# One routing step per slot in the last two heads, its list ahead of the drain's logits, and three output tiles behind the first expert pass

## What is computed

```
attn = softmax(scale * q @ k.T + bias);  x = attn @ v            # (2304, 512)
noisy = x @ w_gate + log1p(exp(x @ w_noise)) * noise             # (2304, 8)
top2, top2_w = best two experts of a token, softmax of their two logits
out[token] = sum over its 2 experts e of  w * (relu(x @ w1[e]) @ w2[e])
```

## Time and profile before

| what | value |
|---|---|
| median of 3 runs | 810.96 us (809.89 to 811.56) |
| the profiled execution | 811.59 us |
| its span, first to last instruction | 809.7 us |
| PE busy | 765.8 us (95%) |
| DVE busy | 495.8 us (61%) |
| ACT busy | 391.5 us (48%) |
| POOL busy | 383.4 us (47%) |
| granted TensorE clock, mean | 0.983 |

### The profile page before, as it was taken

The page is one execution under the profiler, slowest core; times in us unless marked ns, Lnnn a source line. Parts: engine busy times, 40 slices in busy tenths (PEclk is TensorE's granted clock), DMA queues, the critical chain, the costliest instruction groups (busy, mean ns, idle before and its releaser), DMA issues.

```text
span 809.7 us, 18522 instructions
## 1 busy us (share of the span) xinstructions
PE 765.8 (95%) x6658; PEld 623.7 (77%) x6658; DVE 495.8 (61%) x1233; ACT 391.5 (48%) x835; POOL 383.4 (47%) x440
## 2 busy tenths in 40 slices
PE   4886999999999998998999999999999999999994
PEld 2335676776776665978898998998998988988983
DVE  5997898998998897865536335235344344353310
ACT  5996787887887776414324133233232232242200
POOL 0007899899899783063333324314413413423312
PEclk9996999999999999998999999999999999999998
DMA  7785343353353273227633714804804705613112
GB/s 169 214 229 134 107 132 102 104 163 106 107 158 103 87 235 123 63 70 270 189 113 64 204 73 75 253 11 78 260 13 76 249 15 102 221 38 54 39 27 39
DMA packets 51575, 98.49 MB, mean 122 GB/s; under 512 B 12720, under 2 KB 21552, under 8 KB 51504
## 3 DMA queue, kind: packets, MB, share of 16 engines
q1 hardware_dynamic: 39920, 74.55, 29.6%
q0 software_dynamic: 10720, 22.72, 14.0%
q10 hardware_dynamic: 864, 0.29, 0.2%
HBM read 66.38 MB, written 20.53 MB: 107 GB/s over the span
## 4 chain that ended last, share of the span: by engine, by line
PE 80%; DMA 6%; DVE 5%; ACT 3%; issue 3%; POOL 1%; another core or an unknown queue 1%; ACTq 0%; SPq 0%; POOLq 0%; DVEq 0%
PE ps L765 27%; PE po L779 22%; PE po L677 11%; PE ps L595 8%; PE pt L622 6%; DMA out_rows<-ys,iscat 2%; PE pt L601 2%; ACT work L1308 2%; DMA slab<-work 2%; PE pt L636 1%; ACT work L1289 1%; DVE ohlo L1054 1%; PE pt L609 1%; DMA qraw<-in_qT 1%
## 5 line engine op out<-in xcount | busy, mean ns | idle before, releaser
L765 PE MATMUL ps<-xT,whi 128*128 128x320 f32 (+1 forms) x960 | 164.4, 310 | 1.6 <-ACT xT L1458 0.9
L779 PE MATMUL po<-whi,hT 128*128 128x512 f32 x640 | 159.9, 395 | 0.0
L765 PEld LDWEIGHTS ps<-xT,whi 128*128 128x128 f32 x960 | 145.8, 189 | 2.7 <-issue 2.2
L1469 ACT ACTIVATE hT<-ps 128x320 fp32r<-128x320 f32 x112 | 48.8, 437 | 200.8 <-PE ps L765 181.3
L1232 DVE SCALAR_TENSOR_TENSOR hT<-ps,hT 128x320 fp32r<-128x320 f32 x112 | 54.9, 492 | 137.8 <-ACT hT L1469 119.0
L779 PEld LDWEIGHTS po<-whi,hT 128*128 128x128 f32 x640 | 118.2, 188 | 24.6 <-DVE hT L1077 0.5
L1532 POOL TENSOR_SCALAR work<-work,rcp 128x576 f32<-128x576 f32 (+1 forms) x160 | 117.7, 745 | 26.1 <-DVE rcp L947 25.7
L1572 POOL DMA_INDIRECT xg<-x_rows,igath x38 | 42.3, 1112 | 178.5 <-DVE ys L1247 78.8
L934 DVE CUSTOM_DVE_ANT_0 ns<-ps,slab 128x576 f32<-128x576 f32 (+1 forms) x160 | 119.8, 750 | 10.1 <-PE ps L595 6.4
L1324 ACT ACTIVATE work<-ns,nmax 128x576 f32<-128x576 f32 (+1 forms) x160 | 123.1, 769 | 3.9 <-DVE nmax L934 3.8
L1585 POOL DMA_INDIRECT out_rows<-ys,iscat x35 | 60.0, 1713 | 95.4 <-DMA out_rows<-ys,iscat 64.4
(11 more groups left out here) (184 smaller groups left out, 1109.0 us busy)
## 6 DMA issues: line engine op xcount, KB each, us to landing
wraw<-in_mw SPq DMA_DIRECT2D x64, 512.0 KB
slab<-work SPq DMA_DIRECT2D x36, 288.0 KB, 3.8
qraw<-in_qT SPq DMA_DIRECT2D x64, 144.0 KB, 2.8
vs<-in_v SPq DMA_DIRECT2D x32, 160.0 KB, 2.6
out_rows<-zeros SPq DMA_DIRECT2D x32, 152.0 KB
kraw<-in_kT SPq DMA_DIRECT2D x64, 72.0 KB, 2.3
x_rows<-xnat SPq DMA_DIRECT2D x8, 576.0 KB, 4.1
xg<-x_rows,igath POOLq DMA_INDIRECT x38
```

Of the source, the lines that this page charges most:

```text
L765: mm = nc.tensor.matmul(ps[n % 4 // 2][:, n % 2, 0:w], w1s[i][pw][:, c, f * P:(f + 1) * P], x[px][:, c, :], start=j == 0 and c == 0, stop= ...
L779: mm = nc.tensor.matmul(po[:, (i + t) % 2, :], hT[px][:, c, t * P:(t + 1) * P], w2s[i][pw][:, c, :], start=j == 0 and c == 0, stop=j == 2 ...
```

## The change

The early routing moves forward and is spread: `perturbed` in slot 138, `largest` in 139 and 140, `indexed` with three tiles in each of 141 to 144, `first_mask` in 146. TensorE's rank matmuls move from slot 158 to slot `RANK0` = 149. The chain of small operations leaves the drain and stands one to a slot in slots 150 to 159; the ranks are copied out of PSUM first, so that later steps read SBUF. The one-hots stand ahead of the last `recip` and of `evac0(TILES - 6)`, three of them, and nine behind. TensorE makes the list behind `flip(TILES - 4)` and no longer behind the first logits. The three `flip_x` move from among the transposes ahead of the first pass to between its parts j = 0 and j = 1, and ScalarE's three `last_x` behind `xcopy0` and `softplus`.

```diff
@@ -100,6 +100,7 @@
...
 GLAG = OLAG + 1
+RANK0 = OLAG + (B * H - 6) * NU + 2
 FOLD = GLAG + (H - 1) * NU + (B - 2) * H * NU + 2
@@ -671,6 +672,8 @@
...
                         pe.wait_ge(lt_copied, 1)
+                    if n == B * H - 4:
+                        pe.wait_ge(rank0_read, 2)
@@ -715,9 +718,9 @@
...
                     folded(range(CL), po[:, 1, :])
-                if t == TILES - 2:
+                if t == RANK0:
                     pe.wait_ge(mask0_done, 1)
-                    pe.wait_ge(ot_done, B * H - 3)
+                    pe.wait_ge(ot_done, B * H - 5)
                     nc.tensor.matmul(po[:, 0, 0:NEARLY], tri, both[:, 0:NEARLY, 0], start=True, stop=True)
@@ -725,16 +728,15 @@
...
             flip(TILES - 5)
-            pe.wait_ge(rank0_read, 1)
             pv(B * H - 2, (0, 1, 2))
             flip(TILES - 4)
+            pe.wait_ge(ttr_done, TILES)
+            pe.wait_ge(oh0_done, NEARLY + 1)
+            lists(NEARLY, ohlo, oh0, ps[1][:, 1, 0:XB]).then_inc(list0_ready, 1)
             pv(B * H - 2, (3, 4))
             flip(TILES - 3)
-            pe.wait_ge(ttr_done, TILES)
             pe.wait_ge(ot_done, B * H - 2)
             logits(range(H - 2), ps[1][:, 0, :])
-            pe.wait_ge(oh0_done, NEARLY + 1)
-            lists(NEARLY, ohlo, oh0, ps[1][:, 1, 0:XB]).then_inc(list0_ready, 1)
             flip(TILES - 2)
@@ -810,22 +812,21 @@
...
             logits([H - 1], ps[1][:, 0, :]).then_inc(g_ready, 1)
-            flip_x(NX, po[:, 1, :]).then_inc(x_ready, 1)
             pe.wait_ge(g_done, B)
...
             xtr0(2, ps[1][:, 1, :])
-            flip_x(NX + 1, po[:, 0, :]).then_inc(x_ready, 1)
-            for i in range(2):
-                pe.wait_ge(t_done[i], len(ORDER[i]))
-            flip_x(NX + 2, pt[1][:, :]).then_inc(x_ready, 1)
-
             pe.wait_ge(w_hi, W1C)
...
                 if j == 1:
+                    flip_x(NX, po[:, 1, :]).then_inc(x_ready, 1)
+                    flip_x(NX + 1, po[:, 0, :]).then_inc(x_ready, 1)
+                    for i in range(2):
+                        pe.wait_ge(t_done[i], len(ORDER[i]))
+                    flip_x(NX + 2, pt[1][:, :]).then_inc(x_ready, 1)
                     pe.wait_ge(xlo_done, C_XLO + XB)
@@ -1011,23 +1012,50 @@
...
+            early = slice(0, NEARLY)
+
             def early_routing(t):
...
                     copied(range(CL), 0, po[:, 1, :])
-                elif t == FOLD + 4:
+                elif t == FOLD + 3:
                     perturbed(range(CL), 0)
-                elif t in (FOLD + 6, FOLD + 8):
-                    at = (t - FOLD - 6) // 2 * CL
+                elif t in (FOLD + 4, FOLD + 5):
+                    at = (t - FOLD - 4) * CL
                     largest(range(at, at + CL))
-                elif FOLD + 10 <= t < FOLD + 10 + CL:
-                    if t == FOLD + 10:
+                elif FOLD + 6 <= t < FOLD + 10:
+                    if t == FOLD + 6:
                         dve.wait_ge(r_dve, done[0])
-                    indexed(range(2 * (t - FOLD - 10), 2 * (t - FOLD - 9)))
-                elif t == FOLD + 17:
+                    at = (t - FOLD - 6) * NEARLY // 4
+                    indexed(range(at, at + NEARLY // 4))
+                elif t == FOLD + 11:
                     first_mask()
+                elif t == RANK0 + 1:
+                    dve.wait_ge(rank0_ready, 1)
+                    V.tensor_copy(tot[:, 0, early], po[:, 0, NEARLY:2 * NEARLY]).then_inc(rank0_read, 1)
+                    V.tensor_copy(pos[:, early, 0], po[:, 0, early]).then_inc(rank0_read, 1)
+                elif t == RANK0 + 2:
+                    dve.wait_ge(rank0_read, 2)
+                    after(V.tensor_tensor_scan(inc[:, 0, early], ones[:, early], tot[:, 0, early], 0.0, ALU.mult, ALU.add))
+                elif t == RANK0 + 3:
+                    after(V.tensor_tensor(pre[:, 0, early], inc[:, 0, early], tot[:, 0, early], ALU.subtract))
+                elif t == RANK0 + 4:
+                    after(V.tensor_tensor(pos[:, early, 0], pos[:, early, 0], pre[:, 0, early], ALU.add))
+                elif t == RANK0 + 5:
+                    after(V.scalar_tensor_tensor(out=posk[:, early], in0=pos[:, early, 0], scalar=1.0, in1=both[:, early, 0],
+                                                 op0=ALU.add, op1=ALU.mult))
+                elif t == RANK0 + 6:
+                    after(V.tensor_scalar(posk[:, early], posk[:, early], -1.0, None, ALU.add))
+                elif t == RANK0 + 7:
+                    after(V.tensor_copy(poski[:, early], posk[:, early]))
+                elif t == RANK0 + 8:
+                    after(V.tensor_scalar(loi[:, early], poski[:, early], P - 1, None, ALU.bitwise_and))
+                elif t == RANK0 + 9:
+                    after(V.tensor_copy(lof[:, early], loi[:, early]))
+                elif t == RANK0 + 10:
+                    after(V.tensor_tensor(hcol[:, early], posk[:, early], lof[:, early], ALU.subtract))
@@ -1047,7 +1075,6 @@
...
             after_late = range(2 * CL, NT)
-            early = slice(0, NEARLY)
@@ -1086,26 +1113,14 @@
...
             recip(TILES - 2)
-            dve.wait_ge(rank0_ready, 1)
-            after(V.tensor_copy(tot[:, 0, early], po[:, 0, NEARLY:2 * NEARLY]))
-            recip(TILES - 1)
-            after(V.tensor_tensor_scan(inc[:, 0, early], ones[:, early], tot[:, 0, early], 0.0, ALU.mult, ALU.add))
-            after(V.tensor_tensor(pre[:, 0, early], inc[:, 0, early], tot[:, 0, early], ALU.subtract))
-            V.tensor_tensor(pos[:, early, 0], po[:, 0, early], pre[:, 0, early], ALU.add).then_inc(rank0_read, 1)
-            dve.wait_ge(rank0_read, 1)
-            evac0(TILES - 6)
-            after(V.scalar_tensor_tensor(out=posk[:, early], in0=pos[:, early, 0], scalar=1.0, in1=both[:, early, 0],
-                                         op0=ALU.add, op1=ALU.mult))
-            after(V.tensor_scalar(posk[:, early], posk[:, early], -1.0, None, ALU.add))
-            after(V.tensor_copy(poski[:, early], posk[:, early]))
-            after(V.tensor_scalar(loi[:, early], poski[:, early], P - 1, None, ALU.bitwise_and))
-            after(V.tensor_copy(lof[:, early], loi[:, early]))
-            after(V.tensor_tensor(hcol[:, early], posk[:, early], lof[:, early], ALU.subtract))
             dve.wait_ge(consts_done, 5)
...
                 .then_inc(oh0_done, 1)
-            one_hots([(i, 2 * i) for i in range(NEARLY)], oh0_done)
+            one_hots([(i, 2 * i) for i in range(3)], oh0_done)
+            recip(TILES - 1)
+            evac0(TILES - 6)
+            one_hots([(i, 2 * i) for i in range(3, NEARLY)], oh0_done)
             V.tensor_scalar(short[:, :], inc[:, 0, NEARLY - 1:NEARLY], float(HA), float(-HA), ALU.min, ALU.add).then_inc(r_dve, 1)
@@ -1427,12 +1442,12 @@
...
             oevac(B * H - 1)
+            for t, bank in enumerate((ps[0][:, 0, :], ps[0][:, 1, :], ps[1][:, 1, :])):
+                xcopy0(t, bank)
+            softplus(range(CL, NT // 2), 1)
             for half in range(2):
...
             last_x(0, po[:, 1, :])
-            for t, bank in enumerate((ps[0][:, 0, :], ps[0][:, 1, :], ps[1][:, 1, :])):
-                xcopy0(t, bank)
-            softplus(range(CL, NT // 2), 1)
             last_x(1, po[:, 0, :])
```

## The result

The changed kernel takes 816.97 us (median of 6 runs, 815.87 to 819.53) beside 811.35 us for the one before (6 runs, 809.89 to 813.64). The ratio is 1.0072, interval 1.0053 to 1.0091: slower, by 5.6 us in the medians. The forecast was 814.6 us in a range of 809.0 to 817.3. The profiled execution took 816.38 us with a span of 814.5, so the two profiles lie 4.8 us apart, and where they go can be read step by step. A stretch is the distance between two starts on a trace, in us.

What follows compares the result with a forecast made beforehand. TensorE was taken as the bound, with VectorE level in slots 136 to 159. Terms 2.3 - 0.3 + 0.4 + 1.2 = +3.6 us gave 815.2 on the profiled execution, 814.6 on the median; range 809.0 to 817.3.

Steps and rivals of the forecast that it cites:

- A: The loop, ttr(136) to ttr(159): +2.3 us, from -0.5 with nothing held and 2.8 of holds; bounds -2.0 and +3.5.
- The hold of `first_mask`: Slot 146: the comparison sits out GpSimd's split of q, 1.2 us, the addition most of a norm, 0.5.
- The scan's hold: Slot 151: the scan meets GpSimd's next split of q and is held 1.1 us.
- The steps of slots 152 to 158: Loop: six steps meet a norm or split now and then, 0 to 0.2 us each; taken as 0.
- B: From ttr(159) up to flip(TILES - 5): 3.86 us before, -0.3 us predicted; bounds -0.5 and +0.7.
- three of 0.23: Within the stretch up to flip(TILES - 5): three one-hots at 0.23 us each, priced from 2.76 / 12.
- C: The list between the flips: 0.45 us of TensorE's work moved ahead of flip(TILES - 3), +0.4 us; lower bound 0.
- D: To the first pass and beyond: pass 0.7 us earlier, moved flip_x 1.35, VectorE 0.5 more; +1.2 us, bounds -0.7 and +1.5.
- Rival 1: Nothing is held: steps slip between GpSimd's operations; A = -0.5, sum +0.8, 811.8 us; chance 0.23.
- Rival 2: Faster: the loop's TensorE waits go, moved flip_x hide behind a VectorE wait; -2.1, 808.9 us; chance 0.15.
- Rival 3: The 6.88 us stall around the list of all rows, or a loop hold over 3 us, grows; 817.5 us; chance 0.10.
- The signs: Expected in the changed profile: mask comparison and scan over 1 us each, new TensorE waits, gather wait gone, ttr(159) near 307.3.

Runs made afterwards that it cites:

- late_hots: The changed kernel with all twelve one-hots behind the last recip and the evacuation, in place of three ahead; 818.89 us, ratio 1.0071.
- tiny_split: The changed kernel with GpSimd's two splits of head 30 (q and k) cut to 2 columns; 815.08 us, ratio 1.0040.
- flips_back: The changed kernel with the three flip_x and three last_x at their old places; 815.70 us, ratio 1.0054.
- dense_only: The kernel before with only perturbed, largest, indexed and first_mask moved up; rank matmuls and chain stay in the drain; 814.56 us, ratio 1.0037.
- repaired: The changed kernel with first_mask in slot 148 ahead of recip, all one-hots behind the last evacuation, flip_x and last_x at old places; 810.75 us, ratio 0.9999.

## Why the prediction was right, and where it was not

The direction and the mechanism held; the time came out 2.4 us above the forecast, inside the range. Half of that, 1.2 us, is between the profiled executions (815.2 forecast, 816.38 measured), 0.9 of it in the four stretches; the other half is that the medians lie otherwise to the profiled executions than before.

- **A** was 0.6 us too low, and errors of both signs in it partly cancel, so that it came so near is in part luck. The hold of `first_mask` measured 2.6 us (0.2, 1.15 and 1.25 in its three operations) against my 1.7: the addition had to sit out `norm` and the split of k together, where I gave it most of a `norm`. The scan's hold was 0.5 and not 1.1. The steps of slots 152 to 158 (seven, where I wrote six), which I took at 0 with a bound of 1.2, paid some 0.7. With these three my terms would sum to 4.3 us, and not to 3.3; VectorE's busy time grew by 3.4. So the steps themselves were cheaper than the 1.9 I gave them: in slot 153, not held, the evacuation began 0.28 us behind the reciprocal (299.53 to 299.81), beside 0.11 without a step (296.57 to 296.68 before), so a step cost 0.17 and not 0.21. The rest of the difference I can't place. VectorE's idle time shrank by 0.5 where I took 1.0, since new waits of 0.18 and 0.42 us came at the rank copies of slot 150 and right behind them.
- **B** is the step that failed: "three of 0.23". The three one-hots took 1.60 us, because two `norm`s of GpSimd (310.07 to 311.54) began 0.1 us after the first, and the last one-hot ended with them, at 311.59. They have one streamed input, and I had taken their price from a place where GpSimd was idle. The Trainium skill (SBUF — State Buffer, Who interferes with whom) says that a VectorE copy, cast or tensor_scalar can run in a two-port mode and then contends with GpSimd as well. No run shows in which mode the one-hots ran; 1.60 against 0.69 agrees, and late_hots' 3.46 against 2.76. I had quoted that rule and applied it to the small steps of the mask and the chain alone.
- **C** was right: +0.33, the wait at `flip(TILES - 1)` 0.72 where I wrote near 0.8.
- **D** was right in each part. The pass started 0.75 us earlier (0.7). The fifth weight copy began 5.04 us behind it (5.0), VectorE's split 6.14 (6.1), its first `hlow0` 8.91 (8.95). The rows:

```profile
333.49 1.06 ACT L1344 ACTIVATE whi<-wraw 128x1024 fp32r<-128x1024 f32 x1
```

```profile
334.59 1.23 DVE L967 TENSOR_TENSOR wlo<-wraw,whi 128x1024 fp32r<-128x1024 f32 x1 [2.21 <-ACT whi L1344]
...
337.36 1.01 DVE L1104 SCALAR_TENSOR_TENSOR hT<-ps,hT 128x384 fp32r<-128x384 f32 x2
```

  The sum was +0.84 and not +1.2: the three flips took 1.23 of TensorE (331.33 to 332.56), and what VectorE added was 0.4.
- **Rival 1**, nothing held: tiny_split excludes it. **Rival 2**, faster: the flips found no wait to hide in. **Rival 3**: the long stall did not grow. It is 0.87 and 2.09 us in two pieces after, 3.77 before, and that is most of the 0.9 given back. But its clause on a long hold in the loop came half true. TensorE's wait reached 2.79 us, and in some executions the clock fell behind it. The medians differ by 0.8 us more than the profiles do, and I take it that such executions are among the others. The mean granted clock of each points that way, weakly: 0.983 in the profiled one of 816.38 us, 0.978 and 0.981 in the two longest of 818.65 and 819.53, 0.979 to 0.984 in the other three. But a mean over the whole span doesn't say where the clock fell, so this is argued, not shown.
- **The signs.** The mask's comparison, the waits on the gather, at `flip(TILES - 1)`, ahead of the folding and ahead of the first pass came as written. The scan took 0.71 us and not over 1, TensorE's wait near slot 147 was 2.79 us and not 1 to 2.5, and `ttr(159)` started at 308.11 and not near 307.3.

## What to carry to other kernels

Before moving small VectorE steps into a loop, lay GpSimd's timeline beside the slot and look for a long run of operations without a gap: a held step can sit out more than one of them, so moving the mask by two slots was worth 2 us of stretch A here. Put what another engine waits for ahead of the steps that can be held, not behind. Work that stood under a wait is free only there; in a stretch without gaps it costs its full length, and what its successor on a third engine is late by on top.

## What the hardware showed that I had not expected

The same wait of TensorE, 2.79 us in slot 147, had different consequences from execution to execution. The window view after, and of late_hots:

```profile
285.00:290.00 5.00, 2.21 (x38) 1.74 (x36) 4.90 (x12) 1.98 (x6) 3.40 (x4) 1.00 0.62 178
290.00:295.00 5.00, 5.00 (x67) 3.66 (x63) 4.17 (x15) 3.50 (x10) 3.66 (x6) 1.00 0.03 9
```

```profile
285.00:290.00 5.00, 2.21 (x36) 1.78 (x32) 4.86 (x10) 1.92 (x6) 3.85 (x5) 0.87 0.62 173
290.00:295.00 5.00, 5.00 (x44) 3.45 (x40) 2.66 (x8) 2.38 (x6) 2.42 (x4) 0.50 0.04 12
```

TensorE is busy for all of the 5 us in both, but at 1.2 GHz (0.50) it gets 44 matmuls done and not 67. The distance from slot 144 to 149 is 10.10 us after and 12.00 in late_hots. Of the four profiles with the mask in slot 146 and whole splits, three lost the clock (late_hots, flips_back, dense_only) and one didn't. It also fell in repaired after two waits of 0.72 and 0.69 us in the drain, which other executions of the same stretch went through at 1.00:

```profile
314.00:320.00 6.00, 4.59 (x53) 2.48 (x51) 3.25 (x7) 4.29 (x9) 3.26 (x3) 0.93 0.32 89
320.00:326.00 6.00, 5.79 (x35) 3.42 (x32) 2.79 (x4) 1.01 (x2) 0.00 (x0) 0.78 0.16 45
```

flips_back and late_hots run the changed kernel's program in the loop, and their stretch A is 1.4 and 2.4 us longer than its. So the same wait cost its length each time and in some executions one or two us more, and one profile alone doesn't tell its price. What decides between the two no run here shows.
